# Key norms in eight groups instead of six, their pieces placed between other operations of the first bodies

## The reference, cut to what matters

```
k_n = k / (norm(k, axis=-1) + 1e-06)
state = zeros((B, H, D, D))
for t in range(S):
    y[:, :, t] = q[:, :, t] @ state
    v_old = state.T @ k_n[:, :, t]
    state = state + beta_t * outer(k_n[:, :, t], v[:, :, t] - v_old)
```

## Time and profile before

| what | value |
|---|---|
| median of 3 runs | 901.25 us (900.55 to 902.26) |
| profiled execution | 901.16 us |
| span of its profile | 899.4 us |
| PE busy | 834.8 us, 93% of the span |
| DVE, ACT, POOL busy | 65%, 49%, 35% |
| attention, by the last level-opening transpose (L817) | until 370.9 us |

### The profile page before, as it was taken

One profiled execution on the slowest core, in us unless ns is written; L12 is line 12 of the kernel. 1 busy time (PEld: TensorE's weight loads), 2 busy tenths in 40 slices (PEclk: granted clock), 3 DMA queues, 4 the chain that ended last, 5 costly groups with the idle time before them and its releaser, 6 DMA issues.

```text
span 899.4 us, 31660 instructions
## 1 busy us (share of the span) xinstructions
PE 834.8 (93%) x13800; PEld 765.2 (85%) x13800; DVE 583.6 (65%) x1117; ACT 441.8 (49%) x831; POOL 312.0 (35%) x366
## 2 busy tenths in 40 slices
PE   1588999999999999899999999999999999999998
PEld 1466777777877777679999999999999999999997
DVE  6777888888898788656726516436555834646534
ACT  5656777777777667436324124234354433334221
POOL 7566576877676655204100000000022121121210
PEclk9999999999999899989999999999999999999999
DMA  8113212121211110301000000001410100100101
GB/s 275 61 44 102 63 34 63 35 62 33 63 57 40 36 51 20 119 4 54 1 1 1 1 1 0 0 1 62 167 37 0 49 7 1 52 0 0 53 1 54
DMA packets 21648, 38.25 MB, mean 43 GB/s; under 512 B 1808, under 2 KB 15632, under 8 KB 21520
## 3 DMA queue, kind: packets, MB, share of 16 engines
q1 hardware_dynamic: 21520, 36.35, 12.4%
HBM read 31.56 MB, written 4.72 MB: 40 GB/s over the span
## 4 chain that ended last, share of the span: by engine, by line
PE 85%; issue 5%; DVE 4%; ACT 3%; POOL 1%; DMA 1%; SPq 0%; ACTq 0%; POOLq 0%; DVEq 0%
PE dense_ps L1070 16%; PE dense_ps L1072 16%; PE dense_ps L1071 16%; PE t_ps L841 4%; PE front_ps L807 4%; PE z_ps L850 4%; PE t_ps L828 3%; PE t_ps L837 3%; PE front_ps L794 2%; PE side_ps L906 2%; PE side_ps L948 2%; PE extra_ps L960 1%; PE t_ps L817 1%; PE side_ps L931 1%; PE extra_ps L865 1%
## 5 line engine op out<-in xcount | busy, mean ns | idle before, releaser
L1272 POOL TENSOR_TENSOR vn_f<-vn_f 128x384 f32<-128x384 f32 x24 | 24.5, 1022 | 394.1 <-ACT vn_f L1317 394.1
L1070 PE MATMUL dense_ps<-w_spatial_pair,vn_pair 128*128 128x384 f32 x336 | 112.2, 334 | 0.0
L1071 PE MATMUL dense_ps<-w_spatial_pair,vn_pair 128*128 128x384 f32 x336 | 112.2, 334 | 0.0
L1072 PE MATMUL dense_ps<-w_spatial_pair,vn_pair 128*128 128x384 f32 x336 | 112.2, 334 | 0.0
L656 DVE TENSOR_TENSOR w_more<-t_ps,ident_band_lower 64x256 f16<-64x256 f32 x192 | 80.4, 419 | 18.3 <-PE t_ps L828 15.2
L452 ACT ACTIVATE t<-t_ps 128x512 f16<-128x512 f16 (+1 forms) x144 | 60.1, 418 | 44.8 <-PE t_ps L841 42.5
L1513 DVE TENSOR_TENSOR vn_pair<-vn_f,vn_pair 128x384 fp32r<-128x384 f32 x48 | 31.7, 661 | 58.8 <-ACT vn_pair L1279 58.8
L1070 PEld LDWEIGHTS dense_ps<-w_spatial_pair,vn_pair 128*128 128x128 f32 x336 | 63.1, 188 | 0.0
L1072 PEld LDWEIGHTS dense_ps<-w_spatial_pair,vn_pair 128*128 128x128 f32 x336 | 63.1, 188 | 0.0
L1071 PEld LDWEIGHTS dense_ps<-w_spatial_pair,vn_pair 128*128 128x128 f32 x336 | 63.1, 188 | 0.0
L1449 DVE BATCH_NORM_STATS2 stats<-v_u_f 128x6 f32<-128x512 f32 x24 | 16.6, 694 | 62.6 <-ACT v_u_f L1337 62.4
(11 more groups left out here) (229 smaller groups left out, 2650.5 us busy)
## 6 DMA issues: line engine op xcount, KB each, us to landing
qT_in<-in_q SPq DMA_DIRECT2D x24, 256.0 KB, 3.9
k_in<-in_k SPq DMA_DIRECT2D x24, 192.0 KB, 3.1
v_in<-in_v SPq DMA_DIRECT2D x24, 192.0 KB, 2.4
outT<-g_f SPq DMA_DIRECT2D x6, 576.0 KB, 3.2
w_spatial_f<-in_w_spT SPq DMA_DIRECT2D x3, 768.0 KB, 7.3
w_in_f<-in_k SPq DMA_DIRECT2D x2, 960.0 KB, 7.0
x_f<-in_k SPq DMA_DIRECT2D x2, 768.0 KB, 10.3
w_in_f<-in_w_in SPq DMA_DIRECT2D x1, 1536.0 KB, 7.9
```

What stands on the lines that cost most here:

```text
L1070: mm(out, lhs(LO), rhs(HI), start=first, stop=False)
L1071: mm(out, lhs(HI), rhs(LO), start=False, stop=False)
L1072: return mm(out, lhs(HI), rhs(HI), start=False, stop=last)
L1272: tt(ta[:, r], ta[:, r], xt[:, r], ALU.mult).then_inc(zr_full, 1)
```

## The change

The keys' groups become 2, 4 and six times 3 units (eight groups), and the sets become group 0, group 1, and groups 2 to 7. Set 1 then serves units 2 to 5 (32 columns) and set 2 units 6 to 23 (144 columns). `KEPT` is the number of units whose keys lie in the first of the two memories.

The load of group 1 goes ahead of the second key and the first query. POOL makes the two 128x128 identities after the first unit's keys. PE waits only for the small constants at the start, for `halves_in` at its first transposes and for all constants at the first Newton step. POOL waits for each cleared pair by itself. `query(0)` on DVE goes ahead of the clearing of `n_diag`. Each square, sum, root and chain of steps gets a place inside a body: the root is now taken of a quarter of the squares (`scale=0.25`), which lets the six steps be five, and the five of set 2 stand one or two at a time in body 1.

```diff
-GROUPS = ((0, 2), (2, 4), (6, 5), (11, 5), (16, 4), (20, 4))
-NORMS = ((0, 1), (1, 3), (3, 6))
-KEPT = 16
+GROUPS = ((0, 2), (2, 4), (6, 3), (9, 3), (12, 3), (15, 3), (18, 3), (21, 3))
+NORMS = ((0, 1), (1, 2), (2, 8))
+KEPT = 15
 # sync
+            if j == -4:
+                norm_load(1)
             if j == -3:
-                norm_load(1)
+                norm_load(2)
                 ... (halves and masks as before)
-                norm_load(2)
+                norm_load(3)
+                norm_load(4)
             if j == -2:
-                for g in range(3, len(GROUPS)):
+                for g in range(5, len(GROUPS)):
                     norm_load(g)
 # gpsimd
             pool.sem_inc(consts_half, 1)
+        def more_constants():
             for a, one_ in ((negident, -1.0), (identf, 1.0)):
                 ...
-            if u == 0:
-                pool.wait_ge(cleared, 2 + len(knp) + len(kbp))
+            if u < len(knp):
+                pool.wait_ge(cleared, 2 + u + 1)
 ...
             if live(k):
                 key_rests(k)
+            if k == 0:
+                more_constants()
 # scalar: the order in a body; squares 1 and 2 no longer ahead of the bodies
             if live(g):
                 query(g)
+            if g == 0:
+                norm_squares(1)
+            if g == 2:
+                norm_squares(7)
             if live(y):
                 turn(y, 3)
+            if f == 0:
+                norm_squares(3)
             if live(f):
                 n_highs(f)
 ...
                 first_t(f)
+            if g == 0:
+                norm_roots(1)
             if live(g):
                 key_T(g, 0)
+            if x == 0:
+                norm_roots(2)
 ...
             if j == -2:
-                norm_squares(3)
-                norm_squares(4)
-                norm_roots(1)
-                norm_squares(5)
+                norm_squares(2)
             if j == -1:
-                norm_roots(2)
+                norm_squares(4)
+                norm_squares(5)
+                norm_squares(6)
 # vector
+        def norms(i, steps):
+            a, b, h, q = (x[:, norm_columns(i)] for x in (t0, t1, root, squares))
+            ... 0: a = max(h, 1e-18) * 4     1: b = 1 / a      2: a = q * b
+            ... 3: b = (a + 1e-6) + h        4: rnorm = 1 / b
-        norms(0)
+        norms(0, range(5))
 ...
+        query(0)
         for a in nd:
             clear(a[:].rearrange("p h c -> p (h c)"))
         norm_sums(1)
-        norm_sums(2)
 # vector: in a body
             if live(x):
                 level_w(x, 0, 0)
                 level_w(x, 0, C)
+            if x == 1:
+                norms(2, (0, 1))
             ...
                 mask(f, 1)
+            if f == 0:
+                norms(1, range(5))
+            if f == 1:
+                norm_sums(4)
+                norm_sums(5)
             ...
                 level_w(y, 3, C)
+            if y == 0:
+                norms(2, (2,))
             ...
                 mask(f, 0)
+            if f == 2:
+                norms(2, (3,))
             ...
                 level_w(x, 1, C)
+            if x == 1:
+                norms(2, (4,))
             ...
+            if f == 0:
+                norm_sums(2)
+                norm_sums(3)
-            if live(g):
+            if live(g) and g > 0:
                 query(g)
-            if j == -2: norm_sums(3), norm_sums(4)
-            if j == -1: norm_sums(5), norms(1)
-            if j == 0: norms(2)
+            if f == 1:
+                norm_sums(6)
+                norm_sums(7)
 # tensor: waits
-        pe.wait_ge(consts, 1)
-        pe.wait_ge(halves_in, 32)
-        pe.wait_ge(cleared, 2 + len(knp) + len(kbp))
+        pe.wait_ge(consts_half, 1)
         first_t(0):  + pe.wait_ge(halves_in, 32)
         newton(0):   + pe.wait_ge(consts, 1)
```

More of the change, by code:

```diff
@@ L402, in key_rests @@
             tt(n_of[:, 1], kn[:], n_of[:, 0], ALU.subtract).then_inc(kn_rest, 1)
-            if u >= KB:
+            if u < KB:
+                pool.wait_ge(cleared, 2 + len(knp) + u + 1)
+            else:
                 need(pool, s_prod, n_updates(u - KB + 1))
@@ L459, in norm_roots @@
             act.wait_ge(summed, NORMS[i][1])
-            nc.scalar.activation(root[:, norm_columns(i)], squares[:, norm_columns(i)], ACT.Sqrt).then_inc(rooted, 1)
+            nc.scalar.activation(root[:, norm_columns(i)], squares[:, norm_columns(i)], ACT.Sqrt, scale=0.25).then_inc(rooted, 1)
         def clear_w(l):
@@ L552, in scalar @@
         clear_w(4)
-        norm_squares(1)
-        norm_squares(2)
         for j in bodies:
@@ L599, in scalar @@
             if j == -2:
-                norm_squares(3)
+                norm_squares(2)
+            if j == -1:
                 norm_squares(4)
-                norm_roots(1)
                 norm_squares(5)
-            if j == -1:
-                norm_roots(2)
+                norm_squares(6)
     def vector(dve):
@@ L614, in norm_sums @@
                                     squares_of(g).rearrange("p g (h d) -> p (g h) d", h=H), AX.X, ALU.add).then_inc(summed, 1)
[L616 to L631, removed]
+        def norms(i, steps):
+            a, b, h, q = (x[:, norm_columns(i)] for x in (t0, t1, root, squares))
+            for step in steps:
+                if step == 0:
+                    dve.wait_ge(rooted, i + 1)
+                    nc.vector.tensor_scalar(a, h, 1e-18, 4.0, ALU.max, ALU.mult).then_inc(norm_step, 1)
+                if step == 1:
+                    dve.wait_ge(norm_step, 4 * i + 1)
+                    nc.vector.reciprocal(b, a).then_inc(norm_step, 1)
+                if step == 2:
+                    dve.wait_ge(norm_step, 4 * i + 2)
+                    tt(a, q, b, ALU.mult).then_inc(norm_step, 1)
+                if step == 3:
+                    dve.wait_ge(norm_step, 4 * i + 3)
+                    stt(out=b, in0=a, scalar=1e-6, in1=h, op0=ALU.add, op1=ALU.add).then_inc(norm_step, 1)
+                if step == 4:
+                    dve.wait_ge(norm_step, 4 * i + 4)
+                    nc.vector.reciprocal(rnorm[:, norm_columns(i)], b).then_inc(normed, 1)
         def query(u):
@@ L811, in first_t @@
         def first_t(u):
+            if u == 0:
+                pe.wait_ge(halves_in, 32)
             pe.wait_ge(z_first, u + 1)
@@ L854, in newton @@
         def newton(u):
+            if u == 0:
+                pe.wait_ge(consts, 1)
             pe.wait_ge(t_ready[u % 2], turns_of(u, NL - 1))
```

## The result

The changed kernel takes 890.85 us (median of 4 runs, 888.02 to 894.16), the kernel before beside it 901.75 (4 runs, 900.55 to 903.75): a ratio of 0.9878, 95% interval 0.9839 to 0.9917. The forecast was 894.6, with a range from 891.0. A second timing gave 894.05 (6 runs) against 902.77 (17 runs), ratio 0.9897 (0.9857 to 0.9936). So the change is worth 8.7 to 10.9 us by the medians, and the forecast of 6.6 was too small. By how much is less sure: the forecast's ratio, 0.992, lies just outside the first interval, and against the second kernel-before median (0.991) it lies inside the second one.

What follows compares the result with a forecast made beforehand. PE held 85% of the chain, so time is won only where PE waits, with the norms twice in the path. 901.16 less 8.4 before body 1 plus 1.8 lost in it gave 894.6 us, range 891.0 to 899.5.

Steps and rivals of the forecast that it cites:

- part 4: Body 0: two sums replace the six steps at its end; fourth mask at 32.0, body 1 starts at 37.6, not 46.05.
- part 5: Body 1: set 2's five steps cost DVE 3.8 us; body takes 12.0, not 10.25, losing 1.8 (0.8 to 5.2).
- part 6: After body 1: nothing waits for set 2's norms; body 2 on unchanged, units 2 to 23 still 313.4 apart within 1 us.
- Part 1: First key: `kn` starts at 7.5, 2.05 us earlier; `flip(0, 1)` near 10.3, `flip(0, 0)` at 14.35 to 15.4.
- Part 2: Query and group 1: query lands at 10.15, DVE's sum ends at 15.45, first products start at 16.9, not 19.95.
- The low end: First query's landing: 7.98 us as before, instead of the 10.15 taken; `flip(0, 0)` then bounds the first products, at 16.45.
- Part 3: Body -1: first mask at 18.45, 7.2 us earlier, second at 20.8; set 1's five steps, 1.5 to 2, are covered.
- The gain so far: Up to body 1's start: 8.4 us, from 6.1 at `mask(1, 0)` and 2.4 for six steps exchanged for two sums.
- A: Body 1: the port DVE shares with POOL makes all five steps stand in full; 5.2 us lost, 898.0; chance 0.16.
- B: Everything hides: query lands at 7.98, body 1 loses 0.8, PE's high clock comes sooner (about 1); 892.1; chance 0.09.
- C: First bodies: PE's code load meets the key loads, comes 7.0 us late, low clock follows; slower, 903.3; chance 0.07.
- D: No change: the start's gain is given back at something tied to a time, not to the bodies; 901.2; chance 0.06.

Runs made afterwards that it cites:

- win_split: Changed kernel with the one 1536 KB w_in load made into three of 512 KB in bodies 2, 3 and 4: 891.71 us, ratio 0.9883.
- set2_together: Changed kernel with the five steps of set 2 together at the end of body 0 instead of spread in body 1: 902.75 us, ratio 0.9996.
- before_look: Kernel before, no edit, one run more for its profile: 901.37 us.
- before_look2: Kernel before, no edit, a further single run for its profile: 905.80 us.
- before_spread: Kernel before with w_in and w_spatial loads cut into pieces and key and query loads issued apart: 893.82 us, ratio 0.9901.
- before_steps: Kernel before with only its six steps of set 2 moved into body 1, start and groups old: 898.68 us, ratio 0.9968.
- after_again: Changed kernel, no edit, timed again beside the kernel before: 894.05 us, ratio 0.9897.
- after_look: Changed kernel, no edit, one run more for its profile: 885.00 us.
- all_spread: Changed kernel with w_in and w_spatial loads cut into pieces and key and query loads issued apart: 883.60 us, ratio 0.9772.
- big_spread: Changed kernel with w_in loaded as six pieces of 256 KB and w_spatial as six of 384 KB behind later steps: 887.77 us, ratio 0.9833.

## Why the prediction was wrong in size

The measured time came out 3.8 us below the forecast in the first timing and 0.6 in the second. In the profiled pair, whose span was forecast at 892.8 and measured at 888.8, the 4.0 missed divide so: 0.6 up to the start of body 1 (part 4), 0.7 in body 1 (part 5), 2.7 behind it (part 6).

**Part 1, right.** `kn` started at 7.67 (7.5 forecast), `flip(0, 1)` at 10.47 (10.3) and `flip(0, 0)` at 14.86 (14.35).

**Part 2, right.** ACT's copy of the query started at 10.59 (10.15 forecast, so the first query did come behind the 768 KB), DVE's sum ended at 15.72 (15.45), the products started at 17.00 (16.9). The low end had no ground, though: before, the query was issued ahead of group 1 (2.78 and 3.25), so the earlier trace rows do not show a query passing under a load.

**Part 3, right.** First mask at 18.61 (18.45), second at 20.96 (20.8); the five steps of set 1 took 1.8 and were hidden.

**Part 4, right, 0.6 too small.** Third mask 28.72 (28.6), fourth 31.85 (32.0), body 1 at 37.04 (37.6), as the two pairs of sums took 2.6 each and the steps between were a little shorter. The gain so far was 9.0, not 8.4.

**Part 5, the step that failed.** The term is the loss of 1.8 in body 1, 12.0 less 10.25. It took the body 1 of the one profiled execution, 10.25 us with a low stretch of 3.4, as what the change starts from. Both of its sides were off. The five steps took 3.1, not 3.8: the 0.8 charged for POOL beside steps 0 and 1 did not come (0.41 and 1.05). And the body 1 that is replaced takes longer in the other profiles, as PE is low through most of it. By DVE's first level products of body 1 and of body 2 (win_split and set2_together are the changed kernel with one edit each):

| profile | body 1 | takes | of it low |
|---|---|---|---|
| before | 46.05 to 56.30 | 10.25 | 3.4 |
| before_look | 45.51 to 58.33 | 12.82 | 10.2 |
| before_look2 | 45.37 to 58.14 | 12.77 | 10.2 |
| before_spread | 46.23 to 58.67 | 12.44 | 9.8 |
| before_steps | 42.33 to 53.06 | 10.73 | 0 |
| changed kernel, first | 37.04 to 48.39 | 11.35 | 5.1 |
| after_again | 36.56 to 47.31 | 10.75 | 0 |
| after_look | 37.47 to 48.22 | 10.75 | 0 |
| win_split | 36.55 to 49.77 | 13.22 | 11.7 |
| set2_together | 43.91 to 57.04 | 13.13 | 12.2 |

With these, body 1 is no price but a gain. In the mean of three profiles of each kernel it takes 11.9 before and 10.9 after, so 1.0 is gained where 1.8 was to be lost. At unit 2, the mean of three profiles of the kernel before is 58.7 (57.42, 59.44, 59.26) and of three of the changed one 48.8 (49.25, 48.06, 48.96): 9.9, inside the measured 8.7 to 10.9. In the old order DVE waits for PE and the low level lengthens the body; in the changed body, which DVE bounds, 5.1 us of it went with 0.6 more (11.35 against 10.75). I had named the low level in that body, and written that most of it would go; I had not asked whether its length was the same in each execution.

**Part 6, not refuted, but too sure for one profile.** No gain of the change is seen from unit 2 on: before_spread and all_spread have tails of 832.4 and 833.9. But the tail of one and the same program was 834.3, 839.6 and 847.2 in three profiles, with 10.4, 13.8 and 23.9 us of low level in it and stops that sum to 21, 24 and 27. So the sign set for this part, a distance from unit 2 to unit 23 within 1 us of 313.4, can decide nothing: read at the first matmul of unit 23's group it was 312.7 before, and 312.4, 318.4 and 307.0 in the three profiles of the changed kernel. The last 2.4 of the first pair of profiles are of this kind, and a median of 4 runs carries some of it too; the second timing lies inside the range. That the first, 890.85, lies outside it by 0.15 is in part luck; that part 5's term has the wrong sign in the mean of the profiles is not.

**The rivals.** A (the lock on the ports) did not occur in body 1: POOL was idle from 42.57 to 45.29, when the two steps with two inputs stood there (43.18, 44.13). It occurred where the steps stand together (set2_together) and in the kernel before, where a tensor_scalar took 0.80 with 104 columns and 0.20 with 72. This, and not the reciprocal's 0.80 at 41.61 in the earlier trace rows, is what the prediction reads as the lock:

```profile
32.21 0.20 DVE L630 TENSOR_SCALAR x_f<-x_f 128x72 f32<-128x72 f32 x1
...
44.38 0.80 DVE L630 TENSOR_SCALAR x_f<-x_f 128x104 f32<-128x104 f32 x1
```

B came nearest in time. Of its three reasons the query was late and body 1 was not hidden, but the third, PE's clock, is the one that the runs bear out, and it was worth more than the 1 that B gave it. C did not occur: the stops stand at fixed matmuls, 1098 and 10410, and the first code border with a visible stop is matmul 721, at 57.6 us. D is out.

**What the change consists of.** By the place of unit 2, which is 57.4 to 59.4 in the kernel before: the steps alone 53.8 (3.6 to 5.6 earlier), the start and the groups alone (set2_together) 58.2 (0.7 later to 1.3 earlier), both 48.8 (8.7 to 10.7). By time: 3.2, 0.0, and 8.7 to 10.9. The parts have one profile each. The two are worth more together than added, as a start that is 7 us earlier only leads PE into a longer wait and keeps it at the low clock while the steps stand together.

## What to carry to other kernels

Small dependent steps of a side job belong one by one into the gaps of the engine that carries them; together they stop TensorE, and the clock it then loses is paid on top of the steps (body 1 took 12.4 to 12.8 behind them in three profiles, and 10.7 with them inside). Before a stretch's duration is used in a forecast, look whether it holds a low-clock stretch, and put its length in as a range: one profile is one draw. When code streams in behind data, cut large loads into pieces and issue them apart; here that gave 9.0 us in the kernel before (902.85 to 893.82, timed together) and 7 to 10 in the changed one, for no change in the work.

## What the runs showed of the hardware that was not expected

PE's stops without a cause in the profile stand at fixed places of its program: matmuls 721, 1098, 1978, 2481, 3362, 3865 and so on. Count everything that PE's records hold, that is matmuls, weight loads and the waits and register operations between them: from the stop before 721 to the one before 1098 these are 768, and 1024 from 1978 to 2481. All 358 stops of over 0.3 us in the 14 profiles stand an exact multiple of 256 such instructions apart. The Trainium skill (Runtime: NRT & Kernel Launch, Instruction fetch mechanics) has code refilled in blocks of 256 instructions; the trace agrees. The page of the changed kernel has a queue for instructions beside the one for data, with 104 packets of 16 KB:

```profile
q1 hardware_dynamic: 21552, 36.35, 12.4%
q8 instruction: 104, 1.70, 0.8%
```

The packets' own times show the cause that rival C and theory P only argued. Each of the 358 stops ends 2.2 to 3.5 us (median 2.5) after the start of such a packet. Matmul 1098 starts 2.2 to 2.5 us after one in all 14 profiles, and only the packet's place differs: in the changed kernel's three profiles it starts 0.2 to 0.3 us after PE has run dry (69.96, with PE dry from 69.66, in the first), in big_spread 1.4 us and in all_spread 2.1 us before that. So PE does wait for its code there. Cutting the loads under which the two longest stood took these from 2.4 to 3.1 us in the changed kernel to 0.9 or less. Why a packet starts late beside a large load the records do not say.

The rise of the clock in the first bodies differs between executions of the same first 30 us: 35.6, 36.6 and 42.2 us in three profiles of the changed kernel, 48.2 in win_split, where it cost body 1 1.8 to 2.4 more (unit 1 to 2: 14.5, against 12.1 to 12.6). One profile alone shows this for the changed order.

What stays open is the difference in mean clock over the runs, 0.983 before and 0.989 changed. A low stretch of 6.8 us takes half of that, 3.4 us, from the clock, or 0.004 of a span of 900; one of 10.2 us (as in before_spread) takes 0.006. So the low stretch in the old body 1 is about large enough to be all of it. But the low stretches of the later bodies move so much between the few profiles that another part is not excluded.
